# Linear attention and two gated layers on one core: sums of down ahead of step 1, zeros behind the first raw output, one sum of x on GpSimd

## What is computed

```python
kv = einsum('bhsd,bhse->bhde', k, v)           # batch 4, heads 8, seq 576, dim 64
out = einsum('bhsd,bhde->bhse', q, kv)
x = out / sqrt(mean(out * out, -1) + 1e-6) * g_norm       # 2304 tokens x 512
h = x @ w_in;  x = (h * sigmoid(1.702 * h)) @ w_out       # 512 -> 2048 -> 512
h = x @ w_in2; y = log(1 + exp(h)) @ w_out2
```

## Time and profile before

| | |
|---|---|
| median of three executions | 817.9 us |
| profiled execution | 818.39 us |
| its span, first to last instruction | 816.6 us |
| mean granted clock of TensorE | 0.998 |
| TensorE busy (matmul) | 805.2 us, 99% |
| VectorE busy | 588.9 us, 72% |
| ScalarE busy | 425.0 us, 52% |
| GpSimd busy | 223.0 us, 27% |
| longest chain of waits, by engine | PE 92%, DVE 3%, ACT 2% |

### The profile page before, as it was taken

How to read it: one execution, slowest core, us unless ns; L and a number is a source line. 1 busy time by engine, 2 the same in 40 slices (tenths; PEclk the granted TensorE clock), 3 DMA queues, 4 the chain that set the end, 5 groups by cost and what they waited for, 6 DMA issues and landing times.

```text
span 816.6 us, 12377 instructions
## 1 busy us (share of the span) xinstructions
PE 805.2 (99%) x4604; PEld 734.2 (90%) x4604; DVE 588.9 (72%) x1029; ACT 425.0 (52%) x809; POOL 223.0 (27%) x263
## 2 busy tenths in 40 slices
PE   8989999999999999999999999999999999999998
PEld 7978999999999999999998888898888988989886
DVE  3779767687665786665678777888767889766774
ACT  3773332334221233223246776788767678766765
POOL 4888987304421403254501401100000000000000
PEclk9999999999999999999999999999999999999999
DMA  9936547426455462756642525224433322452402
GB/s 358 405 158 236 213 143 280 159 116 217 159 219 203 154 238 91 246 200 250 231 171 101 206 102 205 107 90 150 164 126 119 152 91 101 159 180 90 149 33 77
DMA packets 24426, 139.78 MB, mean 171 GB/s; under 512 B 2224, under 2 KB 6960, under 8 KB 17200
## 3 DMA queue, kind: packets, MB, share of 16 engines
q1 hardware_dynamic: 24224, 138.95, 46.6%
q10 hardware_dynamic: 144, 0.07, 0.0%
HBM read 104.92 MB, written 34.08 MB: 170 GB/s over the span
## 4 chain that ended last, share of the span: by engine, by line
PE 92%; DVE 3%; ACT 2%; issue 1%; DMA 1%; SPq 0%; ACTq 0%; DVEq 0%
PE ps L640 42%; PE ps L705 23%; PE ps L713 16%; PE ps L710 8%; PE ps L583 1%; DMA kv_in_sb<-k_v 1%; PE ps L566 1%; DVE xs_f L984 1%; DVE gs_f L1013 1%; PE ps L602 0%; DVE ex L1066 0%; DVE rms L953 0%; PE ps L588 0%; DVE gs_f L1069 0%; ACT fix L819 0%
## 5 line engine op out<-in xcount | busy, mean ns | idle before, releaser
L640 PE MATMUL ps<-xs,w_in 128*128 128x384 f32 x2016 | 409.5, 338 | 2.3 <-DVE gs_f L1013 2.0
L640 PEld LDWEIGHTS ps<-xs,w_in 128*128 128x128 f32 x2016 | 356.4, 188 | 27.7 <-issue 4.0
L705 PE MATMUL ps<-w_out,gs 128*128 128x512 f32 x864 | 226.0, 393 | 0.0
L1013 DVE TENSOR_TENSOR gs_f<-ps,gs_f 128x384 f32<-128x384 f32 x240 | 133.2, 555 | 113.7 <-PE ps L640 112.2
L705 PEld LDWEIGHTS ps<-w_out,gs 128*128 128x128 f32 x864 | 160.0, 188 | 23.9 <-issue 0.5
L713 PE MATMUL ps<-gs,w_out 128*128 128x512 f32 x576 | 148.2, 392 | 0.0
L713 PEld LDWEIGHTS ps<-gs,w_out 128*128 128x128 f32 x576 | 105.6, 188 | 16.4
L809 ACT ACTIVATE lg<-gs_f 128x384 f32<-128x384 f32 x73 | 38.3, 526 | 123.2 <-DVE gs_f L1013 122.1
L487 POOL TENSOR_TENSOR w_in<-w_in_f,w_in 128x256 fp32r<-128x256 f32 x112 | 94.1, 876 | 29.1 <-ACT w_in L849 28.9
L844 ACT CAST gs<-gs_f 128x384 fp32r<-128x384 f32 x96 | 48.9, 509 | 67.7 <-DVE gs_f L1073 66.4
L710 PE MATMUL ps<-gs,w_out 128*128 128x256 f32 x576 | 83.9, 281 | 0.1
(11 more groups left out here) (64 smaller groups left out, 576.8 us busy)
## 6 DMA issues: line engine op xcount, KB each, us to landing
w_in<-w_kept SPq DMA_DIRECT2D x40, 1792.0 KB, 7.3
w_kept<-w_in SPq DMA_DIRECT2D x16, 1792.0 KB, 10.8
w_in_f<-w_in SPq DMA_DIRECT2D x16, 512.0 KB, 4.1
w_out_f<-w_out SPq DMA_DIRECT2D x16, 512.0 KB, 9.0
kv_in_sb<-k_v SPq DMA_DIRECT2D x8, 640.0 KB, 10.2
kv_in_sb<-k_v SPq DMA_DIRECT2D x8, 576.0 KB, 11.9
q_sb<-q_t SPq DMA_DIRECT2D x16, 288.0 KB, 10.2
out<-xy SPq DMA_DIRECT2D x18, 256.0 KB, 7.8
```

The lines of the kernel that those rows point to most:

```text
L640: mm = nc.tensor.matmul(ps[:, bank, 0:HALF], w[:, wp, W_OF[k], cols], xs[:, k, xp, t], start=(new and t == 0 and (wp, xp) == (HI, HI)), st ...
L705: mm = nc.tensor.matmul(ps[:, acc_bank(1, j), 0:DM], g[:, j * P:(j + 1) * P], w, start=new, stop=done)
L1013: nc.vector.tensor_tensor(to, bank, other, ALU.add).then_inc(added, 1)
```

## The change

It has these parts:

1. TensorE: five products of zeros behind the raw output of unit 0; `down(0, 0, 9)` is issued ahead of step 1's P1 instead of behind it.
2. SyncE: the raw w of step 1 is loaded at unit 6 instead of 5.
3. GpSimd: B21 is split ahead of the sums of step 1's w; the sum T3 is made on GpSimd, behind that w's low parts; the order of the splits becomes B11, B21, B22, T1, T3, T2, T4.
4. VectorE: T1 is made behind the scaling of unit 8 (it needs six x), T2 behind unit 10 and a wait for GpSimd's T3, T4 behind unit 11.
5. Step 0's tail: ScalarE makes C21's sigmoid ahead of the last unit's x; VectorE multiplies and splits C21 ahead of the addition for C12.

```diff
--- before.py
+++ after.py
@@ -151,6 +151,7 @@
         x_hi_early = sem("x_hi_early")
         x_split_early = sem("x_split_early")
         x_raw_made = sem("x_raw_made")
+        t3_early = sem("t3_early")
         x_hi_made = sem("x_hi_made")
         x_split = sem("x_split")
 
@@ -268,7 +269,9 @@
         X_SPLIT_ORDER = (B11, T2, B21, T3, T4, T1, B22)
         X_RAW_ORDER = (T3, T2, T4, T1)
 
-        X_EARLY = (B11, B21, B22, T3, T2, T4, T1)
+
+        X_EARLY = (B11, B21, B22, T1, T3, T2, T4)
+        X_EARLY_SUMS = (T1, T2, T4)
 
 
 
@@ -300,7 +303,10 @@
             return x_block(ci, 0, 1), x_block(ci, 0, 0), ALU.subtract
 
         def x_raws(ci, slot):
-            return 4 * ci + X_RAW_ORDER.index(slot) + 1
+
+            if ci == 0:
+                return X_EARLY_SUMS.index(slot) + 1
+            return len(X_EARLY_SUMS) + 4 * (ci - 1) + X_RAW_ORDER.index(slot) + 1
 
         def x_his(ci, slot):
             return 7 * (ci - 1) + (X_HI_ORDER if ci < X_LATE_FROM else X_LATE_ORDER).index(slot) + 1
@@ -428,7 +434,7 @@
                 sp.dma_start(out[row:row + P, :].rearrange("p (a n) -> p a n", a=2), tile_rows(ci, j)
                              ).then_inc(stored, 16)
 
-            W_AT = {0: 0, 5: 1, 11: 2}
+            W_AT = {0: 0, 6: 1, 11: 2}
             load_kv(0)
             for u in range(UNITS):
                 if u + 1 < UNITS:
@@ -506,6 +512,11 @@
                                                 w_out[:, f, HI, cols].bitcast(F32), ALU.subtract
                                                 ).then_inc(w_out_split, 1)
 
+            def first_t3():
+                pool.wait_ge(x_made, 2 * PAIRS)
+                a, b, op = x_sum_of(0, T3)
+                nc.gpsimd.tensor_tensor(x_sum(0, T3), a, b, op).then_inc(t3_early, 1)
+
             def x_early(slot):
 
                 if slot in X_RAW_ORDER:
@@ -524,10 +535,12 @@
             w_high(0)
             w_low(0)
             x_early(B11)
+            x_early(B21)
             w_sums(1)
-            x_early(B21)
             w_high(1)
             w_low(1)
+
+            first_t3()
             for slot in X_EARLY[2:]:
                 x_early(slot)
             w_out_low(0, 0)
@@ -656,6 +669,9 @@
                 if u + 1 < UNITS:
                     kv_product(u + 1)
                 raw_output(u)
+                if u == 0:
+
+                    zeros(5)
                 if u >= TURN_LAG:
                     turn(u - TURN_LAG)
                 if u == P1_UNIT:
@@ -733,8 +749,10 @@
             product(0, P5)
             turn(UNITS - 1)
             product(0, P3)
+
+            down(0, 0, shares(1)[P1])
             for m in range(1, ALL):
-                came = 0
+                came = shares(1)[P1] if m == 1 else 0
                 for k in range(PRODUCTS):
                     product(m, k)
                     down(m - 1, came, shares(m)[k])
@@ -827,6 +845,8 @@
                 if u == UNITS:
                     nc.scalar.preload_act_table_set("sigmoid_and_others")
                     hidden(0, C11)
+                if u == UNITS + 1:
+                    hidden(0, C21)
                 if u >= TURN_LAG:
                     gain(u - TURN_LAG)
 
@@ -914,7 +934,8 @@
                     round_x(ci + 1, T3)
                 if ends_late:
                     round_x(ci + 1, T3)
-                hidden(m, C21)
+                if m > 0:
+                    hidden(m, C21)
                 if ends:
                     round_x(ci + 1, T2)
                     round_x(ci + 1, T4)
@@ -976,7 +997,9 @@
                     dve.wait_ge(w_stored, 16 * 2 * STEPS)
                 if ci > X_LATE_FROM:
                     dve.wait_ge(x_split, x_splits(ci - 1, T1))
-                if slot == T2:
+                if slot == T2 and ci == 0:
+                    dve.wait_ge(t3_early, 1)
+                elif slot == T2:
                     dve.wait_ge(x_raw_made, x_raws(ci, T3))
                 if slot == T4:
                     dve.wait_ge(x_raw_made, x_raws(ci, T2))
@@ -1019,14 +1042,14 @@
                 if u == UNITS - 1:
                     add(0, U3)
                 scale(u)
-                if u == 2 * PAIRS + 1:
-                    dve.wait_ge(x_made, 2 * PAIRS)
-                    raw_x(0, T3)
+                if u == 2 * PAIRS:
+
+                    dve.wait_ge(x_made, PAIRS + 2)
+                    raw_x(0, T1)
+                if u == 2 * PAIRS + 2:
                     raw_x(0, T2)
-                if u == 2 * PAIRS + 2:
+                if u == 2 * PAIRS + 3:
                     raw_x(0, T4)
-                if u == 2 * PAIRS + 3:
-                    raw_x(0, T1)
 
             def copy_sums(ci):
 
@@ -1132,19 +1155,13 @@
                 add(m, C22_ADD)
                 if m == 0:
                     gate_split(m, C11)
-                    add(m, C12_ADD)
                 if phase:
                     softplus(m, C21)
                 else:
-                    gate_product(m, C21)
-                    if m > 0:
-                        gate_split(m, C21)
-                if m > 0:
-                    add(m, C12_ADD)
+                    gate(m, C21)
+                add(m, C12_ADD)
                 if ends:
                     low_x(ci + 1, T2)
-                if m == 0:
-                    gate_split(m, C21)
                 if ends_late:
                     low_x(ci + 1, T3)
                 if p == 0 and ci >= CHUNKS:
```

## The result

The changed kernel takes **820.58 us** (median of 11 executions, 819.93 to 821.56), the kernel before 818.47 (11 executions, 817.61 to 818.86). The ratio is 1.0026, with a 95% interval of 1.0018 to 1.0034: 0.26% or 2.1 us slower. The profiled execution took 819.93 us, with a span of 818.0 us (816.6 before).

A forecast was written before the change was run, and what follows sets the result against it. TensorE, busy 99% of the span, bounds the kernel. An early gain of 0.6 us is hidden by GpSimd's late T2; P6 and then the whole shift 1.1 us, so 817.9 + 1.1 = 819.0 us, range 816.4 to 821.2.

The forecast's parts named there:

- rival (a): Clock falls to half behind a gap before P6 or down: one fall, chance 0.26, 820.4; both gaps, 0.07, 821.8.
- the forecast's way: GpSimd's late T2 starts P6 1.1 us later, and TensorE shifts as a whole: 819.0 at full clock.
- The zeros and the transfers: First gap near 10 us: zeros keep full clock, worth 1.7 us, but k and v transfers limit the gain to 0.6.
- GpSimd: More work ahead of T2's split and three pushes of 0.74 by VectorE's sums: T2 ready at 51.9, P6 1.1 later.
- rival (b): VectorE and GpSimd do not push each other: P6 starts at 49.8, total 816.8 down to 816.2; chance 0.24.
- TensorE up to P6: Most waits in line 583 go; TensorE reaches P6 near 48.5, then waits some 3 us for GpSimd.
- a clock that stays up: Behind the first gap, up to 10.54 us: zeros filling 1.4 of 1.69 us keep full clock, which would give 1.7.
- From P6 to step 1: Step 0's tail: TensorE waits 1.5 us or more before down; down and P1 end at 65.65, 64.52 before.
- Behind it TensorE is full and shifts as a whole: After step 0's tail, TensorE has no slack, so the delay of 1.1 us carries through to the end.

The follow-up runs named there:

- e8: The kernel before the change, with only the five products of zeros behind unit 0's raw output added: 818.49 us, ratio 1.0002.
- e4: The changed kernel, with the sum T3 made on VectorE again, behind unit 9: 819.94 us, ratio 1.0019.
- e11: The changed kernel with small matmuls that move nothing in both gaps, nine ahead of P6 and seven ahead of down: 819.42 us, ratio 1.0017.
- e3: The changed kernel, with step 1's raw w loaded at unit 5 and summed ahead of B21's split, as before the change: 817.98 us, ratio 0.9997.
- e5: e3 with GpSimd's sums of the third w moved behind its wait for C21's split: 818.22 us, ratio 1.0004.
- e1: The changed kernel with nine small matmuls that move nothing in the gap ahead of P6: 821.14 us, ratio 1.0036.
- e9: e5 with step 1's low parts of w_out ahead of the fourth w's sums, and ScalarE's rounding of that w later: 820.90 us, ratio 1.0035.
- e12: e3 with seven small matmuls that move nothing in the gap ahead of down's first sums: 817.13 us, ratio 0.9991.
- e10: e9 with GpSimd's splits in the order B11, B21, B22, T3, T2, T4, T1: 821.06 us, ratio 1.0035.
- e6: The changed kernel with its fifth part (the reordered tail of step 0) undone: 819.86 us, ratio 1.0021.
- e2: The changed kernel, with only GpSimd's split of T1 moved from fourth place to last: 819.03 us, ratio 1.0011.
- e7: The kernel before, with the change's fifth part (the reordered tail of step 0) alone: 818.25 us, ratio 1.0003.

## Why the prediction was right or wrong

It forecast no change that can be told (819.0 us, 1.1 us slower), with a chance of 0.38 for slower by more than 0.2%. Measured was 2.1 us slower (0.26%), inside the range of 816.4 to 821.2, and by the mechanism of rival (a), priced at 820.4: the forecast's way for 1.1 to 1.6 us, and one stretch at half clock on top. The kernel before had meanwhile come out at 818.47 and not 817.9, which makes 0.6 us of the distance between 819.0 and 820.58. That 820.58 lies so near rival (a)'s 820.4 owes something to this.

- **The zeros and the transfers**: right in kind. The clock stays up at 11 us. P1 of step 0 came 0.45 us earlier where 0.6 was said, with TensorE waiting for unit 8's k and v at 26.34 as foretold. The wait of 0.81 us for q at 16.65 was not foretold; the prediction had said that no wait would be left in that line (583 before, 596 now). That the zeros alone did not lower the median of the kernel before (e8) was not foreseen either.
- **GpSimd**: right. T2 at 51.58 (51.9 forecast), P6 at 51.64 (52.0), 0.7 us later than before instead of 1.1. The pushes were 0.72, 0.61 and 0.60 us instead of three times 0.74, and struck second halves and w's low parts, not casts. In e4 all four of VectorE's sums pushed GpSimd, three of them a cast by 0.73 us. So rival (b) falls. The exclusive lock that the Trainium skill (SBUF — State Buffer, section "Who interferes with whom") describes agrees with that. But the prediction's reading of it, that each sum pushes GpSimd by its own length, does not hold: T4's sum took 0.95 us, 0.74 of it beside the second half that it met (from 43.86 on), and pushed by 0.60.
- **TensorE up to P6**: right. Its last work ahead of P6 ended at 48.80, where "near 48.5" was said, and the gap was 2.83 us, where some 3 was said.
- **The step that failed** is the one that was not taken: "a clock that stays up" was weighed for the first gap only, and the sum was then made as if the clock were full behind a gap of 3 us, while the trace of before showed half clock behind one of 1.69 us. That case was given 0.26 for one fall. In the changed kernel it came in all eleven executions. Its price, forecast as 1.4, measured 0.7 to 1.2 (e11, by the ratios and by the medians), and 1.0 to 1.6 inside one kernel (e3, e4, e5).
- **From P6 to step 1**: the forecast of 1.5 us or more of waiting before down, with VectorE's split and product both pushed, is what e1 (2.00), e3 (1.98) and e11 (1.72 of filler and 0.45) show, with 0.97 and 1.07 us in VectorE's row. In the changed kernel itself the half clock had slowed TensorE, VectorE met less of GpSimd, and the wait was 1.04. So a fall at the first gap is partly given back at the second, and repairing the first alone (e1) sends the fall to the second. The rivals treated the two gaps as two independent losses; they are not. In the profiled execution the two errors largely cancel: P7 came at 56.23 and not 55.45, down's wait was 1.04 us and not 1.5 or more, and step 1's P6 began at 65.88, where 65.65 was forecast. That this sum came out so near was luck.
- **"Behind it TensorE is full and shifts as a whole"** held for the changed kernel, whose waits beyond 66 us are those of before. It does not hold for kernels that run ahead: in e5 and e9 GpSimd's later work took the gain back.

## What to carry to other kernels

When work is moved off one helper engine onto another, sum up what the second must finish before each deadline of the main engine, holes included: here a sum of 1.8 us, a split put first (2.7), a hole of 2.35 and pushes of 1.9, less 3.0 us in which GpSimd had stood idle on the way and 0.7 by which it now began earlier, made one operand some 5 us later (51.58 against 46.77), and only 4.2 us of that had been slack. Price every gap that a change opens in TensorE's row twice, once as a wait and once as a chance of half clock behind it; if gaps must be there, cheap matmuls in them held the clock here (e8, e11, e12), but all the gaps of some 2 us had to be filled, not the first alone.

## What the runs showed that was not expected

The clock as a matter of chance: the kernel before has two kinds of executions, with and without a stretch at half clock behind its gap of 1.69 us (12 of 27, 10 of 32, 5 of 17 and 5 of 15 with one), 0.4 to 0.7 us apart. With a longest gap, as profiled, of 2.96 us it was 5 of 5 (e9) and 5 of 6 (e10), of 2.93 us 8 of 10 (e6), of 2.83 us 11 of 11 (the changed kernel), of 2.74 us 10 of 11 (e2), of 2.0 us 4 of 5 (e1), 6 of 11 (e4) and 4 of 11 (e3), of 1.78 us 3 of 11 (e5), of 1.69 us 4 of 11 (e7), and with the gap of 1.69 or those of 2 us and more filled none of 33 (e8, e11, e12). One median therefore mixes two times, and a change that moves a gap changes the mixture.
